# One compare moved from VectorE to GpSimd, and the exps, normalisations and transposes around it put in another order, in a fused top-k attention and gated product

## The reference

```python
# q, k, v: (4, 8, 576, 64) float32; w_a, w_b: (512, 1536); w_out: (1536, 512)
scores = np.matmul(q, k.transpose(0, 1, 3, 2)) / np.sqrt(64)
kth = np.partition(scores, -32, axis=-1)[..., -32:-31]
scores = np.where(scores >= kth, scores, -1e9)
attn = np.exp(scores - scores.max(-1, keepdims=True))
attn = attn / (attn.sum(-1, keepdims=True) + 1e-9)
x = np.matmul(attn, v).transpose(0, 2, 1, 3).reshape(4 * 576, 512)
out = ((x @ w_a) * (x @ w_b)) @ w_out
```

## Time and profile before

| | |
|---|---|
| median of 3 runs | 903.66 us (903.11 to 904.3) |
| the profiled execution | 903.46 us |
| its span, first to last instruction | 901.7 us |
| outside the span | 1.8 us |
| busy share PE, DVE, ACT, POOL | 92%, 86%, 68%, 52% |
| granted TensorE clock, mean | 0.964 of full speed |

### The profile page before, as it was taken

The page is one execution under the profiler, slowest core; times in us unless marked ns, Lnnn a source line. Parts: engine busy times, 40 slices in busy tenths (PEclk is TensorE's granted clock), DMA queues, the critical chain, the costliest instruction groups (busy, mean ns, idle before and its releaser), DMA issues.

```text
span 901.7 us, 19246 instructions
## 1 busy us (share of the span) xinstructions
PE 830.7 (92%) x6664; PEld 744.1 (83%) x6664; DVE 777.1 (86%) x1668; ACT 614.2 (68%) x1328; POOL 472.4 (52%) x561
## 2 busy tenths in 40 slices
PE   4467678999999999999999999999999999999998
PEld 3355557998899999888999999888999998998897
DVE  3689999997989999989899999988999999997000
ACT  3577777777776777777777776786677777776322
POOL 1667764456545554565454555555454555555232
PEclk9985659999999999999999999999999999999999
DMA  4424651223352232233432322243333222321332
GB/s 111 122 91 131 200 183 52 83 61 87 92 126 66 66 98 74 66 89 94 110 82 76 98 66 65 66 110 86 92 84 102 70 66 71 93 62 54 100 96 75
DMA packets 133008, 81.48 MB, mean 90 GB/s; under 512 B 82224, under 2 KB 109872, under 8 KB 132912
## 3 DMA queue, kind: packets, MB, share of 16 engines
q1 hardware_dynamic: 132368, 80.12, 32.0%
q10 hardware_dynamic: 544, 0.13, 0.1%
HBM read 70.78 MB, written 9.44 MB: 89 GB/s over the span
## 4 chain that ended last, share of the span: by engine, by line
PE 62%; DVE 26%; issue 5%; ACT 4%; DMA 1%; POOL 1%; SPq 1%; ACTq 0%; POOLq 0%
PE ps L473 25%; PE ps L486 13%; DVE work L787 12%; DVE best L770 10%; PE ps L404 6%; PE ps L414 6%; PE ps L437 5%; DVE keep L802 3%; PE ps L363 3%; PE ps L376 2%; ACT k_t L543 1%; DMA k_rows<-in_k 1%; PE ps L429 1%; PE ps L384 1%; ACT scores L580 1%
## 5 line engine op out<-in xcount | busy, mean ns | idle before, releaser
L770 DVE MAX8 best<-work 128x8 f32<-128x576 f32 x432 | 316.7, 803 | 0.0
L707 POOL TENSOR_TENSOR scores<-scores,keep 128x576 f32<-128x576 f32 x144 | 216.4, 1523 | 89.9 <-DVE keep L802 89.9
L473 PE MATMUL ps<-x_hi,w_hi 128*128 128x256 f32 x864 | 250.4, 290 | 1.1 <-ACT x_lo L597 1.1
L473 PE MATMUL ps<-x_lo,w_hi 128*128 128x256 f32 x864 | 243.2, 282 | 0.0
L787 DVE MATCH_REPLACE8 work<-best,work 128x576 f32<-128x576 f32 x288 | 222.7, 798 | 0.0
L473 PE MATMUL ps<-x_hi,w_lo 128*128 128x256 f32 x648 | 182.7, 282 | 0.0
L473 PEld LDWEIGHTS ps<-x_hi,w_hi 128*128 128x128 f32 x864 | 162.8, 188 | 2.9 <-ACT x_lo L597 2.0
L473 PEld LDWEIGHTS ps<-x_lo,w_hi 128*128 128x128 f32 x864 | 162.9, 189 | 0.5
L717 POOL TENSOR_TENSOR h_lo<-ab,h_hi 128x256 fp32r<-128x256 f32 x108 | 79.7, 738 | 128.7 <-ACT h_hi L608 128.6
L572 ACT ACTIVATE scores<-scores,neg_max 128x576 f32<-128x576 f32 x144 | 112.1, 779 | 46.7 <-POOL scores L707 46.6
L713 POOL TENSOR_TENSOR ab<-ab 128x256 f32<-128x256 f32 x108 | 80.1, 742 | 114.1 <-ACT ab L603 111.6
(11 more groups left out here) (52 smaller groups left out, 1331.3 us busy)
## 6 DMA issues: line engine op xcount, KB each, us to landing
wo_lo<-x_scratch SPq DMA_DIRECT2D x108, 256.0 KB, 2.8
wb_lo<-x_scratch SPq DMA_DIRECT2D x108, 128.0 KB, 2.2
stage<-in_w SPq DMA_DIRECT2D x36, 256.0 KB, 2.7
q_rows<-in_q SPq DMA_DIRECT2D x142, 64.0 KB, 2.2
x_scratch<-wo_lo SPq DMA_DIRECT2D x18, 256.0 KB, 2.4
k_rows<-in_k SPq DMA_DIRECT2D x32, 128.0 KB, 2.4
v_rows<-in_v SPq DMA_DIRECT2D x32, 128.0 KB, 2.6
out<-stage SPq DMA_DIRECT2D x15, 256.0 KB, 2.6
```

The source lines that it names most:

```text
L473: last = mm(ps_ab[:, which, :], w, x[:, g % 2, kb, :], start=(kb == 0 and i == 0), stop=(kb == KB - 1 and i == 2))
L707: V.tensor_tensor(row, row, keep[:, j, :], ALU.add).then_inc(mask_done, 1)
L770: ins = V.max(best[:, u % 2, j, 8 * r:8 * r + 8], src)
```

## The change

`below` of tile 1 leaves VectorE and goes to GpSimd, between the two additions `masked`. On ScalarE the exponent of tile 1 moves behind the second half of x and q, both normalisations are put together behind `between(s, 2)`, the copy of the transposed tile 0 comes behind `between(s, 3)`, and that of tile 1 goes to the head of the next slot. On TensorE the transposes of tile 0 move behind `steps(todo[3])`, and those of tile 1 to the head of the next slot. VectorE's `invert` moves from the second to the third round.

```diff
@@ TensorE
             for s in range(FIRST, LAST):
                 todo = steps_of(s)
+                transposes(s - 2, 1)
                 steps(todo[0])
                 probs_v(s - 2)
                 q_transposes(s + 2)
...
                 steps(todo[2])
-                wait(pe, qt_ready, min(s + 3, NU))
                 if s in PREP_AT:
                     k_transposes(PREPS.index(PREP_AT[s]), 1)
+                steps(todo[3])
+                wait(pe, qt_ready, min(s + 3, NU))
                 wait(pe, kt_ready, 2 + 2 * sum(at <= s for at in PREP_AT if at >= FIRST))
                 transposes(s - 1, 0)
-                steps(todo[3])
-                transposes(s - 1, 1)
                 steps(todo[4])
@@ ScalarE
             for s in range(FIRST, LAST):
+                copy_probs_t(s - 2, 1)
                 if s in PREP_AT:
                     split_k(PREPS.index(PREP_AT[s]))
                 between(s, 0)
                 exps(s - 1, 0)
                 x_out(s - 2, x_hi, pv_done, xhi_done)
-                exps(s - 1, 1)
                 copy_q(s + 2, 0)
                 copy_scores(s + 1, 0)
                 between(s, 1)
-                normalise(s - 1, 0)
                 x_out(s - 2, x_lo, xsub_done, xlo_done)
                 copy_q(s + 2, 1)
+                exps(s - 1, 1)
                 copy_scores(s + 1, 1)
                 if s in PREP_AT:
                     copy_k(PREPS.index(PREP_AT[s]), 0)
-                normalise(s - 1, 1)
                 between(s, 2)
                 if s in PREP_AT:
                     copy_k(PREPS.index(PREP_AT[s]), 1)
+                normalise(s - 1, 0)
+                normalise(s - 1, 1)
+                between(s, 3)
                 copy_probs_t(s - 1, 0)
-                between(s, 3)
-                copy_probs_t(s - 1, 1)
                 between(s, 4)
@@ GpSimd
+            def below(u, j):
+                if not unit(u):
+                    return
+                pool.wait_ge(kth_ready, 2 * u + j + 1)
+                wait(pool, mask_done, 2 * (u - 1) + j + 1)
+                V.tensor_scalar(keep[:, j, :], scores[:, u % ROWS, j, 0:S], best[:, u % 2, j, TOPK - 1:TOPK], NEG,
+                                ALU.is_lt, ALU.mult).then_inc(keep_ready[j], 1)
...
                 masked(s - 1, 0)
+                below(s - 1, 1)
                 masked(s - 1, 1)
@@ VectorE
                 take_out(s, 1, 0)
-                invert(s - 1)
                 take_out(s, 1, 1)
                 find(s, 2)
+                invert(s - 1)
                 take_out(s, 2, 0)
                 take_out(s, 2, 1)
                 find(s, 3)
                 below(s, 0)
-                below(s, 1)
             invert(NU - 1)
```

## The result

| | before | after |
|---|---|---|
| median | 903.45 us (903.11 to 904.3, 4 runs) | 956.72 us (955.96 to 957.9, 4 runs) |
| profiled execution, its span | 903.46, 901.7 us | 957.9, 956.1 us |

The ratio is 1.059, with a 95% interval of 1.057 to 1.061: slower by 53 us, where 28 were forecast and 946 was the top of the range. The direction and several of the waits were right, the size was not.

The account below looks back on a forecast made before the run. VectorE was taken as the bound in plain slots, by 2% over TensorE. Plain pairs +17, last-unit pairs +5, k pairs -3, slots 3 to 8 +8, slots 9, 10 and ends +1: +28 on 903.46, 931 us; range 908 to 946.

Parts of the forecast that it names:

- VectorE's relief: Compare off VectorE saves 0.42 us a slot, to 10.13; TensorE's need then limits a plain pair to 20.7 us.
- The wait on the PSUM region: Four-step slots: tile 1's transposes, back to back with tile 0's, wait for its copy, taken as 1.25 us, some 30 times.
- the walk: Step-by-step timing of a four-step slot from x_subtract: first normalisation at about 2.95 us, TensorE ready at 3.96, wait 1.13.
- TensorE isn't held: Four-step slot: the first normalisation ends at 3.73 us, before TensorE can begin tile 0's transposes at 3.96; no wait.
- I take 0: Five-step slot: the first normalisation ends about when TensorE arrives, so no added time.
- the ring: Slots that split weights: loop from one first normalisation to the next, 12.5 us a slot against 11.17.
- the cost on the path nothing: GpSimd's added compare, taken as 1.0 us and at most 1.6, is covered by over 1 us before tile 1's exponent.
- six pairs with k: Pairs that transpose k: 2.5 us back, 1.25 and about 0.75 more taken; -0.5 each, -3 us together.
- Rival C: GpSimd's compare takes over 3 us, making the second mask late for the exponent; 4 us would give about 1000; chance 0.05.
- The early slots: Slots 3 to 8, which split weights: six slots lengthen by 8 us together.
- plain pairs: Slots 11 to 70: 20 pairs of plain slots go from 21.10 to 21.95 us, 0.85 each, +17 us.
- My top of 946: Upper end of the range: stall of 1.5 us, k pairs giving nothing back, early ring a bit longer.

Follow-up runs that it names:

- e3: The kernel before with tile 1's compare left out, tile 1 masked with tile 0's keep: 892.6 us.
- e9: The changed kernel with the compare back on VectorE and a PSUM place of its own for tile 1's transposes: 907.0 us.
- e6: The changed kernel with a PSUM place of its own for tile 1's five transposed blocks: 946.2 us.
- e8: The changed kernel with the compare back on VectorE and both normalisations ahead of between(s, 2): 925.2 us.
- e1: The changed kernel with tile 1's compare back on VectorE, the new order kept: 948.5 us.
- e10: The changed kernel with the compare back on VectorE, tile 1's own PSUM place and both normalisations ahead of between(s, 2): 910.0 us.
- e11: The changed kernel with GpSimd's compare as one operation, without the multiply, so tile 1 is not masked: 951.1 us.
- e7: The changed kernel with tile 1's own PSUM place and both normalisations ahead of between(s, 2), compare still on GpSimd: 962.7 us.

## Why the prediction was wrong in size

**VectorE's relief** (10.13 us a slot, TensorE's need 20.7 a pair): right. e3 measured 10.13 in five-step slots and 20.74 a pair.

**The wait on the PSUM region**: right, 30 times. In the changed kernel tile 0's transposes start at 790.10, and tile 1's at 791.71; less 0.47 for issuing five, that is 1.14 us, where the walk gave 1.13 and I took 1.25. e9 prices it at 1.10 a pair. In a plain pair of the changed kernel itself taking it away gives nothing, since the loop over GpSimd holds that slot (e6).

**"TensorE isn't held" by the normalisation, and "I take 0" for the five-step slot**: the first step that failed. Both slots:

```profile
778.52 0.74 PE L414 MATMUL ps<-ident,scores 128*128 128x128 f32 x5 [0.24 <-ACT scores L580]
...
790.10 0.74 PE L414 MATMUL ps<-ident,scores 128*128 128x128 f32 x5 [0.31 <-ACT scores L580]
```

The walk had ScalarE right to 0.1 us: normalisation 0 starts at 789.07, 3.04 us after `x_subtract` at 786.03, and I had 2.95. But TensorE was placed too late. From the earlier trace rows I took 0.92 us to the first step, 1.53 for it and 1.51 for the second, where transposes stand between the two; back to back, as the change puts them, it is 0.75, 1.43 and 1.42 (786.78, 788.21, about 789.63), so TensorE comes at 3.6, not 3.96. And from the end of a normalisation to the transposes it takes 0.25 us (789.84 to 790.10), for which the walk had nothing. Neither slot is free: 0.47 and 0.33 us of wait. e8 prices the two together at 0.81 a pair. With 1.10 that is 1.9 us a pair, against my 1.25, and 20.75 + 1.9 gives the 22.7 that e1 shows. This is what TensorE loses, not what there is to win: with both edits the pair is 21.69 (e10), 1.0 less than e1's, because the chain over exponent 1 holds the slot of four steps at 11.1. For the plain slots the forecast walked half of that chain and never closed it from `invert` to `invert`; in the early slots it did, as the ring, and there it was right.

**The compare on GpSimd, "the cost on the path nothing"**: the second one. The size was outside my bounds, 2.22 us for 1.0 and at most 1.6. And the path was another: I looked for the exponent that waits for the mask, and had even seen that the product's multiply stands behind other work on GpSimd, but only in the slot of four steps. In the slot of five the multiply stands behind both masks and the compare. The loop is 11.69 us long and binds in that slot, so that the changed kernel's pair is this loop and the third chain, 11.7 and 11.0 to 11.2; the compare costs 8 us by e1, mostly in slots 9 and 10 (23.6 to 21.7 us) and in those with k (slots 31 to 35, 63.5 to 61.6), which is part of why six pairs with k came out longer and not 0.5 shorter each: in the stretches 14 to 19, 30 to 35 and 48 to 53 the changed kernel is 7.5 us over the kernel before, and 2.9 of them remain in e1. Rival C had the compare as the danger, from 3 us on and by way of the mask; at 2.22 it bit, at 1.73 (e11) no longer in plain slots. The estimate of about 0.5 us that stands beside my 1.0 in the prediction was further off still.

**The early slots**: +8 forecast, +8.0 measured, and the ring of 12.5 (its first part adds up to 9.1, not 9.2) is 12.51. The mechanism was right too: in the slot of the changed kernel that normalises at 96.85, ScalarE works without a gap from the score copy at 93.57 on, 3.28 us where the walk had 3.4, in the order that it gives; and the compare has no part in it, since e1 takes 75.1 us there as well.

In the sum: plain pairs +1.7 instead of +0.85 each, 17 us more for 20 of them; the others with the k slots, 6 or 7 more; slots 9, 10 and ends, 3 more. My top of 946 had a stall of 1.5 us, no wait for the normalisation and no loop over GpSimd.

## What to carry to other kernels

When a wait is taken away and the time stays, look for a loop of nearly the same length before the wait is called harmless: here three edits gave 2, 10 and -6 us with the second loop in place, and two of them 23 and 41 without it; both together gave 38, and behind them stood a third loop. When work is moved to an engine with air, list everything that stands behind it in that engine's queue in every kind of slot, not only its own consumer. Where a change has one good part (here the step between k's transposes and the tile's), try it alone: with a PSUM place of its own it gave 1.1% where the whole cost 5.9%.

## What was not expected of the hardware

GpSimd's TENSOR_SCALAR of 128 x 576 with a compare against a value per row and a multiply took 2.22 us, 1.73 without the multiply; the two-input addition of the same size on the same engine took 1.42. From start to start the three are 2.30, 1.81 and 1.52 us. One input less didn't make it shorter. VectorE's compare of that size lasts 0.50 us and costs 0.42 from start to start. ScalarE's normalisation to TensorE's next transposes took 0.25 us, while ScalarE's copy out of PSUM to the transposes behind it took 0.14. In e7 an idle stretch of TensorE of 1.44 us was followed by the lower clock in some slots and not in others, and where it was, the slot took 1.6 us longer (12.67 for 11.10).
